# Fused attention and two-layer networks on one core: value means spread by ScalarE, a load queue that holds loads alone

## The chip, the cores and the metric

The kernel runs on one core of a Trainium2 chip. The metric is device time in microseconds (us) of one execution. Five engines run their own instruction streams beside each other and meet at semaphores: PE (TensorE, matmuls), DVE (VectorE), ACT (ScalarE), POOL (GpSimd) and SP (SyncE, which here only issues DMAs). Sixteen DMA engines move the data.

## The reference

```python
def _attn_ref(q, k, v):                      # B, H, S, D = 2, 8, 768, 64
    block, window = (32, 16)
    k_sum = k.reshape(B, H, nb, block, D).max(axis=3)
    v_sum = v.reshape(B, H, nb, block, D).mean(axis=3)
    scores_l = scale * q @ k^T, kept where |i - j| < window
    scores_s = scale * q @ k_sum^T + np.log(block)
    a = softmax(concatenate([scores_l, scores_s]))
    return a @ concatenate([v, v_sum])

def _moe_ref(x, w_in, w_out):                # 1536 tokens, 512 -> 2048 -> 512
    h = np.maximum(x @ w_in, 0.0)
    return h * h @ w_out

def _moe2_ref(x, w_in, w_out, a, b):
    h = x @ w_in
    g = (a[0] + a[1]*h + a[2]*h*h + a[3]*h*h*h) / (1.0 + |b[0]|*|h| + |b[1]|*h*h + 1e-06)
    return g @ w_out
```

Each query sees a band of 31 keys around itself and, beside them, one summary per block of 32 keys (the maximum of the keys, the mean of the values). The attention output is the input of a first network, and that one's output the input of a second.

## The kernel before

**The attention** works on eight units n = 0 to 7 (NB), each a pair of heads of one batch entry, called a head here for short. A head has 12 windows of 64 queries, done in three groups of four windows, so there are 24 groups G = 0 to 23 (GROUPS), and head n has groups 3n, 3n+1, 3n+2. For a group, PE computes the scores (`scores`, L483) against the windowed keys `kwin`; DVE adds the mask and takes the extreme (`masked`, L833, tile `prob`, `lowest`); ACT does four exponentials (`exps`, L665); DVE inverts the sums; POOL scales (`normalise`, L381); PE transposes (`turn`, L502, into bank 6); ACT copies the transposed matrix to `probT` (L687); PE multiplies with the values (`output`, L519). Scores run four groups ahead of the output, exponentials three.

**Loads per head:** queries `q` (384 KB), keys `kraw` (384 KB), windowed values `vwin` (two halves of 288 KB). DVE takes block maxima of the keys (`block_max`, L818) and POOL copies keys into windows (L351). `q`, `kraw` and `kwin` have rings of three buffers (RING), `vwin` of four (V_RING).

**Value means.** PE multiplies the values with a matrix of 1/32 (`summary(n)`, L493) in the group given by `SUMMARY_AT[n]`, ACT copies the result to `vsum` (`copy_summary`, L673), and four DMAs of 36 KB each (`spread_summary`, L262) copy the 24 means behind the 96 value rows of each of the 12 windows of `vwin`: each DMA writes 6 partitions x 12 windows of 512 B. `output(3n)` waits for all four (`vsum_in`). These DMAs read and write SBUF only.

**The queue.** Before, all loads and all spreads are issued by SP, in one written order, and each instruction that waits holds up all behind it. A load of head n+3 waits until its buffer is free; a spread waits for `vsum_copied`, that is for ACT's copy of that head's means.

**The networks** follow. PE runs them without a pause once the attention has ended: L533 (first product) and L585, L600 (second products). The weights come through `wraw` (512 KB each): three during the attention (`load_first`, split into high and low parts by POOL), the others later (`load_weights`, L272, split by DVE).

Of the kernel before, what the change touches and what calls it, by code (L numbers as in the profile page):

```python
# [28 lines left out]
P = 128  # L29
# [4 lines left out]
KW = QW + 2 * BAND  # L34
NW = S // QW
NBLK = S // BLOCK
COLS = KW + NBLK
GU = 4
GPB = NW // GU
# [9 lines left out]
FT = DF // P  # L49
# [4 lines left out]
EARLY = PAIRS - 1  # L54
# [6 lines left out]
P_RING = 4  # L61
RING = 3
V_RING = 4
NB = PAIRS * B
# [1 line left out]
KP = S + 2 * BAND  # L66
THIRD = S // GPB
SPLIT_FROM = GROUPS - 7
SUMMARY_AT = [0, 1, 3] + [GPB * n - 4 for n in range(3, NB)]


def unit(j, h):
# [4 lines left out]
def done(credits, i):  # L77

    return credits + i + 1


def build(nc, qT, kT, vw, w1, w2, coef_a, coef_b, out):
# [33 lines left out]
    ca = small("ca", [P, 4])  # L116
    braw = small("braw", [P, 2])
# [8 lines left out]
    q, kraw, kwin, vwin = [], [], [], []  # L126
# [101 lines left out]
    def landing(index, k=0):  # L228

        return (index - EARLY) % LAND, k + (index - EARLY) // LAND  # L230
# [5 lines left out]
    def _(sp):  # L236
        def load_k(n):
            if n >= RING:
                sp.wait_ge(windows_ready, GPB * (n - RING + 1))
            sp.dma_start(kraw[n % RING][:, BAND:BAND + S], kT[n]).then_inc(k_in[n % RING], 16)  # L240
# [5 lines left out]
        def load_q(n):  # L246
            if n >= RING:
                sp.wait_ge(s_done, GPB * (n - RING + 1))
            sp.dma_start(q[n % RING][:, :], qT[n]).then_inc(q_in[n % RING], 16)

        def load_vwin(n):
            if n >= V_RING:
                sp.wait_ge(o_done, done(2, GPB * (n - V_RING + 1) - 1))
            for half in (slice(0, NW // 2), slice(NW // 2, NW)):
                sp.dma_start(vwin[n % V_RING][0:KW, half, :], vw[n][:, half, :]).then_inc(vw_in[n % V_RING], 16)

        def spread_summary(n):

            sp.wait_ge(vsum_copied, n + 1)
            for t in range(4):  # L260
                rows = KW + 2 * GPB * t
                sp.dma_start(vwin[n % V_RING][rows:rows + 2 * GPB, :, :],  # L262
                             vsum[n % 2][32 * t:32 * t + 2 * GPB, :].unsqueeze(1).to_broadcast([2 * GPB, NW, P])
                             ).then_inc(vsum_in[n % V_RING], 16)

        def load_first(j):
            sp.dma_start(wraw[:, j:j + 1, :], w1[j:j + 1].rearrange("a p n -> p a n")).then_inc(w_first, 16)

        def load_weights(w, j, index, turn):
            if not (isinstance(turn, int) and turn == 0):  # L270
                sp.wait_ge(w_in[index], 16 * turn)
            sp.dma_start(wraw[:, bass.ds(j, 1), :], w[bass.ds(j, 1)].rearrange("a p n -> p a n")).then_inc(w_in[index], 16)  # L272

        load_k_first(0)
        load_k_first(2)
        load_q(0)
        load_vwin(0)
        load_k(1)
        load_q(1)
        load_k(2)  # L280
        load_vwin(1)
        load_q(2)
        for n in range(NB):
            if n == 0:
                load_vwin(2)
            elif n + RING < NB:
                load_vwin(n + RING)
            if n + RING < NB:
                load_k(n + RING)
            if n == 0:  # L290
                spread_summary(0)
                load_vwin(RING)
                spread_summary(1)
            if n + RING < NB:
                load_q(n + RING)
            if 2 <= n < 2 + EARLY:
                load_first(n - 2)
            if n == 5:
                sp.dma_start(ca[:, :], coef_a.partition_broadcast(P)).then_inc(coef_in, 16)
                sp.dma_start(braw[:, :], coef_b.partition_broadcast(P)).then_inc(coef_in, 16)  # L300
            if n >= 5:
                for j in range(EARLY + 2 * (n - 5), min(EARLY + 2 * (n - 4), FT // 2)):
                    load_weights(w1, j, *landing(j))
            if n == 1:
                spread_summary(2)
            if 0 < n and n + 2 < NB:
                spread_summary(n + 2)
        sp.wait_ge(o_done, done(2, GROUPS - 1))
        with sp.Fori(0, FT // 2 // LAND) as k:
            for i in range(LAND):  # L310
# [333 lines left out]
    def _(act):  # L644
# [13 lines left out]
            last = a.copy(means[:, j, 2 * j:2 * j + 2], mean[:, :])  # L658
        last.then_inc(means_done, 1)

        def exps(G, r):

            act.wait_ge(s_free, done(2, G))
            for u in range(GU):
                last = a.activation(prob[r][:, u, :], prob[r][:, u, :], ACT.Exp, bias=lowest[r][:, u:u + 1],  # L665
                                    scale=-1.0, accum_out=rowsum[r][:, u:u + 1])
            last.then_inc(exp_done, 1)

        def copy_summary(n):
            act.wait_ge(vsum_done, n + 1)  # L670
# [9 lines left out]
        exps(0, 0)  # L680
        exps(1, 1)
        copy_summary(0)
        exps(2, 2)
        for G in range(GROUPS):
            act.wait_ge(t_done, done(P_RING, G))
            act.wait_ge(o_done, done(2, G - 2))
            a.copy(probT[G % 2][:, :], tps[0:COLS, :]).then_inc(probT_done, 1)  # L687
            if G + 3 < GROUPS:
                exps(G + 3, (G + 3) % P_RING)
            if G == GROUPS - 2:  # L690
                relu(0, 0)
            for n in range(1, NB):
                if SUMMARY_AT[n] == G:
                    copy_summary(n)
# [352 lines left out]
```

## Time and profile before

| | |
|---|---|
| median of 3 runs | 622.24 us (619.99 to 626.68) |
| profiled execution, its own time | 619.3 us |
| its span, first to last instruction | 617.2 us |
| granted TensorE clock | 0.999 |
| last attention matmul (L519 of group 23) starts | 85.44 us |
| busy: PE, DVE, ACT, POOL | 94%, 72%, 42%, 24% of the span |

Times in the views are us from the start of the span. The span less 85.44 us is the networks, in which PE is busy throughout; the attention is the stretch ahead of it. The profiled execution's own time is 2.1 us over its span.

### The profile page before, as it was taken

The numbers are of one execution on the slowest core, as the hardware profiler recorded it, in microseconds if no ns is written. First come the engines' busy times: TensorE is split into PE (matmuls) and PEld (weight loads), VectorE is DVE, ScalarE is ACT, GpSimd is POOL, SyncE is SP. The second block draws the span as 40 slices with busy tenths as digits, with TensorE's granted clock in tenths as the row PEclk, the third lists the DMA queues.
The fourth block names the chain that finished last, engine by engine and source line by source line (L and its number), as shares of the span: only waits on it lengthen the run. The fifth ranks groups of instructions, "written<-read, shape, count | busy, mean of one in ns | idle before, by whom it ended". The sixth has DMA issues, their size and how long they took to land.

```text
span 617.2 us, 9768 instructions
## 1 busy us (share of the span) xinstructions
PE 581.2 (94%) x3360; PEld 473.0 (77%) x3360; DVE 443.0 (72%) x839; ACT 261.6 (42%) x556; POOL 147.2 (24%) x158
## 2 busy tenths in 40 slices
PE   4587899999999999999999989999999999999995
PEld 3465678888888888888888867788888888888884
DVE  5467798765343333356765699999999999999996
ACT  4477731110131110311110855566766566766564
POOL 6255640000030000120000566622222222222220
PEclk9999999999999999999999999999999999999999
DMA  8477544000000000023322200000100000100001
GB/s 252 100 212 246 191 163 184 0 1 0 1 1 0 0 0 0 0 68 103 103 102 102 69 1 0 1 0 1 68 0 0 0 0 0 69 1 0 1 1 68
DMA packets 13535, 32.55 MB, mean 53 GB/s; under 512 B 1728, under 2 KB 4416, under 8 KB 13504
## 3 DMA queue, kind: packets, MB, share of 16 engines
q1 hardware_dynamic: 13360, 31.99, 16.1%
q8 instruction: 21, 0.34, 0.2%
q10 hardware_dynamic: 144, 0.13, 0.1%
q14 instruction: 10, 0.08, 0.0%
HBM read 27.79 MB, written 3.15 MB: 50 GB/s over the span
## 4 chain that ended last, share of the span: by engine, by line
PE 46%; DVE 35%; issue 9%; ACT 3%; DMA 3%; SPq 2%; DVEq 1%; POOL 0%; POOLq 0%
PE bank L533 22%; PE bank L585 21%; DVE ratio L981 9%; DVE numer L963 6%; DVE ratio L975 5%; DVE numer L961 5%; DVE ratio L970 5%; DVE hhi L988 4%; DMA kraw<-kT 3%; ACT prob L665 2%; SPq L262 1%; PE bank L502 1%; PE bank L519 1%; DVE hlo L992 1%; PE bank L483 1%
## 5 line engine op out<-in xcount | busy, mean ns | idle before, releaser
L533 PE MATMUL bank<-xhi,whi 128*128 (+1 forms) x384 | 149.8, 390 | 0.1
L533 PE MATMUL bank<-xhi,wlo 128*128 (+1 forms) x384 | 149.4, 389 | 0.0
L533 PE MATMUL bank<-xlo,whi 128*128 (+1 forms) x384 | 149.4, 389 | 0.0
L443 POOL TENSOR_TENSOR denom<-denom,habs 128x512 f32<-128x512 f32 (+1 forms) x49 | 62.3, 1273 | 251.0 <-ACT denom L736 251.0
L678 ACT ACTIVATE hsq<-bank 128x512 f32<-128x512 f32 x48 | 28.8, 600 | 213.2 <-PE bank L533 213.1
L533 PEld LDWEIGHTS bank<-xhi,whi 128*128 128x128 f32 x384 | 72.1, 188 | 15.2 <-issue 0.3
L533 PEld LDWEIGHTS bank<-xhi,wlo 128*128 128x128 f32 x384 | 72.1, 188 | 15.1
L533 PEld LDWEIGHTS bank<-xlo,whi 128*128 128x128 f32 x384 | 72.1, 188 | 14.7
L600 PE MATMUL bank<-whi,hhi 128*128 128x512 f32 x192 | 75.9, 395 | 7.6 <-DVE hlo L992 7.6
L600 PE MATMUL bank<-wlo,hhi 128*128 128x512 f32 x192 | 74.8, 390 | 0.0
L600 PE MATMUL bank<-whi,hlo 128*128 128x512 f32 x192 | 74.8, 390 | 0.0
L585 PE MATMUL bank<-hhi,whi 128*128 128x512 f32 x192 | 74.7, 389 | 0.0
L585 PE MATMUL bank<-hlo,whi 128*128 128x512 f32 x192 | 74.7, 389 | 0.0
L585 PE MATMUL bank<-hhi,wlo 128*128 128x512 f32 x192 | 74.7, 389 | 0.0
L875 DVE TENSOR_TENSOR hsq<-hsq 128x512 f32<-128x512 f32 x48 | 33.4, 697 | 49.8 <-ACT hsq L678 49.8
L878 DVE TENSOR_SCALAR hhi<-hsq 128x512 fp32r<-128x512 f32 x48 | 21.1, 439 | 64.2 <-PE bank L585 64.1
L981 DVE SCALAR_TENSOR_TENSOR ratio<-numer,ca,ratio 128x512 f32<-128x512 f32 (+1 forms) x49 | 56.7, 1158 | 5.7
L435 POOL TENSOR_TENSOR xlo<-xraw,xhi 128x512 fp32r<-128x512 f32 x12 | 17.4, 1483 | 169.9 <-ACT xraw L713 169.9
L733 ACT ACTIVATE habs<-bank 128x512 f32<-128x512 f32 x48 | 28.8, 599 | 66.9 <-PE bank L533 51.6
L600 PEld LDWEIGHTS bank<-whi,hhi 128*128 128x128 f32 x192 | 36.0, 188 | 19.1 <-DVE hlo L992 11.8
L744 ACT ACTIVATE bank<-denom,one 128x512 f32<-128x512 f32 (+1 forms) x49 | 33.6, 686 | 32.4 <-POOL denom L443 32.4
L992 DVE TENSOR_TENSOR hlo<-ratio,hhi 128x512 fp32r<-128x512 f32 (+1 forms) x49 | 42.0, 858 | 1.7
(69 smaller groups left out, 862.2 us busy)
## 6 DMA issues: line engine op xcount, KB each, us to landing
wraw<-w SPq DMA_DIRECT2D x32, 512.0 KB, 4.1
vwin<-vw SPq DMA_DIRECT2D x16, 288.0 KB, 5.4
q<-qT SPq DMA_DIRECT2D x8, 384.0 KB, 6.0
out<-osb SPq DMA_DIRECT2D x12, 256.0 KB, 2.1
kraw<-kT SPq DMA_DIRECT2D x7, 384.0 KB, 6.1
vwin<-vsum SPq DMA_DIRECT2D x32, 36.0 KB
kraw<-kT SPq DMA_DIRECT2D x2, 128.0 KB, 2.4
kraw<-kT ACTq DMA_DIRECT2D x1, 128.0 KB, 2.7
```

Source lines behind the costliest of these rows:

```text
L443: g.tensor_tensor(denom[:, i, cols], denom[:, i, cols], habs[:, i, cols], ALU.mult).then_inc(q_done, 1)
L533: last = mm(hps[j % 2][:, :], W[a][:, j, kt * P:(kt + 1) * P], X[b][:, kt, bass.ds(CH * c, CH)], start=kt == 0 and i == 0, stop=kt == KT - ...
L585: last = mm(acc[dt][:, :], W[a][:, j, KT * P + dt * P:KT * P + (dt + 1) * P], HID[b][:, j % 2, :], start=j == 0 and i == 0, stop=j == FT - ...
L600: last = mm(acc[t][:, :], HID[a][:, j % 2, t * P:(t + 1) * P], W[b][:, j, KT * P:], start=j == 0 and i == 0, stop=j == FT - 1 and i == 2)
L744: a.activation(rcp0[bank][:, cols], denom[:, i, cols], ACT.Ln, bias=one[:, 0:1]).then_inc(ln_done, 1)
L875: d.tensor_tensor(hsq[:, i, :], hsq[:, i, :], hsq[:, i, :], ALU.mult).then_inc(sq_done, 1)
L961: d.tensor_tensor(numer[:, i, :], hps[i][:, :], numer[:, i, :], ALU.mult).then_inc(horner_done, 1)
L963: d.scalar_tensor_tensor(numer[:, i, :], numer[:, i, :], ca[:, 1:2], hps[i][:, :], ALU.subtract, ALU.mult).then_inc(h_free, 1)
L970: d.scalar_tensor_tensor(ratio[:, cols], denom[:, i, cols], one[:, 0:1], rcp0[bank][:, cols], ALU.add, ALU.mult).then_inc(t1_done, 1)
L975: d.scalar_tensor_tensor(ratio[:, cols], ratio[:, cols], -2.0, rcp0[bank][:, cols], ALU.add, ALU.mult).then_inc(t2_done, 1)
L981: d.scalar_tensor_tensor(ratio[:, cols], numer[:, i, cols], ca[:, 0:1], ratio[:, cols], ALU.subtract, ALU.mult).then_inc(ratio_done, 1)
L992: d.tensor_tensor(hlo[:, i, cols], ratio[:, cols], hhi[:, i, cols].bitcast(F32), ALU.subtract).then_inc(g_ready, 1)
```

## The change

ACT issues the spreads, one after each of the first exponentials of a group; SP issues loads only. Three things move:

- `spread_summary(n, t)` is now one DMA of ACT. Heads 0, 1 and 2 issue all four in one group of exponentials (head 0 in `exps(2)`, head 1 in those done at G = 2, head 2 at G = 5); heads 3 to 7 issue two at G = SUMMARY_AT[n] + 1 and two a group later. For heads 4 to 7 each issue also waits until the last output of the head that had the buffer is done.
- The SP queue: loads in the order q(n), k(n+1), vwin(n); the first weights behind vwin(3), vwin(4) and vwin(5); the coefficients and five more weights behind vwin(7).
- `SUMMARY_AT[2]` is 4, before 3.

```diff
-SUMMARY_AT = [0, 1, 3] + [GPB * n - 4 for n in range(3, NB)]
+SUMMARY_AT = [0, 1, 4] + [GPB * n - 4 for n in range(3, NB)]
...
         load_q(0)
+        load_k(1)
         load_vwin(0)
-        load_k(1)
-        load_q(1)
-        load_k(2)
-        load_vwin(1)
-        load_q(2)
-        for n in range(NB):
...
+        for n in range(1, NB):
+            load_q(n)
+            if n + 1 < NB:
+                load_k(n + 1)
+            load_vwin(n)
+            if RING <= n < RING + EARLY:
+                load_first(n - RING)
+        sp.dma_start(ca[:, :], coef_a.partition_broadcast(P)).then_inc(coef_in, 16)
+        sp.dma_start(braw[:, :], coef_b.partition_broadcast(P)).then_inc(coef_in, 16)
+        for j in range(EARLY, FT // 2):
+            load_weights(w1, j, *landing(j))
...
-        def exps(G, r):
+        def exps(G, r, spreads=()):
 
             act.wait_ge(s_free, done(2, G))
             for u in range(GU):
                 last = a.activation(prob[r][:, u, :], prob[r][:, u, :], ACT.Exp, bias=lowest[r][:, u:u + 1],
                                     scale=-1.0, accum_out=rowsum[r][:, u:u + 1])
-            last.then_inc(exp_done, 1)
+                if u < len(spreads):
+                    if u == GU - 1:
+                        last.then_inc(exp_done, 1)
+                    spread_summary(*spreads[u])
+            if len(spreads) < GU:
+                last.then_inc(exp_done, 1)
+
+        def spread_summary(n, t):
+
+            act.wait_ge(vsum_copied, n + 1)
+            if n >= V_RING:
+                act.wait_ge(o_done, done(2, GPB * (n - V_RING + 1) - 1))
+            rows = KW + 2 * GPB * t
+            act.dma_start(vwin[n % V_RING][rows:rows + 2 * GPB, :, :],
+                          vsum[n % 2][32 * t:32 * t + 2 * GPB, :].unsqueeze(1).to_broadcast([2 * GPB, NW, P])
+                          ).then_inc(vsum_in[n % V_RING], 16)
...
+            spreads = []
+            for n in range(1, NB):
+                first = SUMMARY_AT[n] + 1
+                if n < RING and G == first:
+                    spreads = [(n, t) for t in range(4)]
+                elif n >= RING and G == first:
+                    spreads = [(n, 0), (n, 1)]
+                elif n >= RING and G == first + 1:
+                    spreads = [(n, 2), (n, 3)]
```

On SP at the start of the program, the order as a difference. A number behind a name tells buffers apart (`kraw0`, `kraw1`, `kraw2` are the ring of keys; `vwin3` is the fourth value buffer):

```order
+L240 DMA kraw1_67<-kT 128x768
 L255 DMA vwin0_65<-vw 96x768 x2
-L240 DMA kraw1_67<-kT 128x768
...
+L240 DMA kraw0_63<-kT 128x768 [waits windows_ready]
 L255 DMA vwin2_73<-vw 96x768 x2
-L240 DMA kraw0_63<-kT 128x768 [waits windows_ready]
-L262 DMA vwin0_65<-vsum0_74 6x12x128 [waits vsum_copied]
-L262 DMA vwin0_65<-vsum0_74 6x12x128 x3
+L249 DMA q0_62<-qT 128x768 [waits s_done]
+L240 DMA kraw1_67<-kT 128x768 [waits windows_ready]
 L255 DMA vwin3_85<-vw 96x768 x2
```

The first spreads have left the queue, and the queries of head 3 and the keys of head 4 stand ahead of the values of head 3; the keys of head 4 came behind the spreads of heads 0 and 1 before.

On ACT, head 3, before:

```order
L673 COPY vsum1_75<-bank7 128x128 [waits vsum_in1,vsum_done]
L687 COPY probT0_83<-bank6 120x512 [waits o_done,t_done]
L665 ACTIVATE prob1_80,rowsum1_97<-prob1_80,lowest1_93 128x120 [waits s_free]
L665 ACTIVATE prob1_80,rowsum1_97<-prob1_80,lowest1_93 128x120 x3
L687 COPY probT1_84<-bank6 120x512 [waits o_done,t_done]
```

and the same place in the changed kernel:

```order
L661 COPY vsum1_75<-bank7 128x128 [waits vsum_in1,vsum_done]
L684 COPY probT0_83<-bank6 120x512 [waits o_done,t_done]
L638 ACTIVATE prob1_80,rowsum1_97<-prob1_80,lowest1_93 128x120 [waits s_free]
L653 DMA vwin3_85<-vsum1_75 6x12x128 [waits vsum_copied]
L638 ACTIVATE prob1_80,rowsum1_97<-prob1_80,lowest1_93 128x120
L653 DMA vwin3_85<-vsum1_75 6x12x128 [waits vsum_copied]
L638 ACTIVATE prob1_80,rowsum1_97<-prob1_80,lowest1_93 128x120 x2
L684 COPY probT1_84<-bank6 120x512 [waits o_done,t_done]
```

Two DMAs now stand between the exponentials, and two more follow in the next group.

## Rows read from the trace of the kernel before

**Rows 1.** Page, part 2: the span in 40 slices, busy tenths of PE and DMA.

```profile
PE   4587899999999999999999989999999999999995
DMA  8477544000000000023322200000100000100001
```

**Rows 2.** Waits of the SP queue, 0 to 140 us: in total, times, longest.

```profile
SPq L262 <- ACT vsum L673: 28.1, 7, 11.0
```

**Rows 3.** The chain that ended last, in order of time: start, us, what.

```profile
14.81 7.23 issue
...
26.50 0.28 ACT vsum L673
...
29.13 3.08 DMA vwin<-vsum
```

**Rows 4.** Timeline of SP: start, us, engine, line, operation.

```profile
7.43 0.40 SPq L240 DMA_DIRECT2D kraw<-kT  x1
11.49 3.27 SPq L262 DMA_DIRECT2D vwin<-vsum  x4
...
26.79 3.06 SPq L262 DMA_DIRECT2D vwin<-vsum  x4
...
31.32 0.43 SPq L240 DMA_DIRECT2D kraw<-kT  x1
...
32.27 8.66 SPq L262 DMA_DIRECT2D vwin<-vsum  x8
...
41.94 0.43 SPq L240 DMA_DIRECT2D kraw<-kT  x1
```

**Rows 5.** Timeline of DVE: the first block maxima of heads 5, 6 and 7.

```profile
47.01 0.42 DVE L818 TENSOR_REDUCE ksum<-kraw 128x8 f32<-128x256 f32 x1 [2.68 <-DMA kraw<-kT]
...
55.40 0.42 DVE L818 TENSOR_REDUCE ksum<-kraw 128x8 f32<-128x256 f32 x1 [2.18 <-DMA kraw<-kT]
...
64.14 0.42 DVE L818 TENSOR_REDUCE ksum<-kraw 128x8 f32<-128x256 f32 x1 [2.55 <-DMA kraw<-kT]
```

**Rows 6.** Timeline of PE: the outputs of groups 0, 3, 6, 18 and 23.

```profile
22.04 1.12 PE L519 MATMUL bank<-probT,vwin 120*64 120x64 f32 x16 [7.23 <-issue]
...
32.34 0.69 PE L519 MATMUL bank<-probT,vwin 120*64 120x64 f32 x16 [1.42 <-DMA vwin<-vsum]
...
39.92 0.69 PE L519 MATMUL bank<-probT,vwin 120*64 120x64 f32 x16 [1.24 <-issue]
...
72.76 0.69 PE L519 MATMUL bank<-probT,vwin 120*64 120x64 f32 x16
...
85.44 0.69 PE L519 MATMUL bank<-probT,vwin 120*64 120x64 f32 x16
```

**Rows 7.** Timeline of ACT, groups 7 to 9.

```profile
41.23 0.59 ACT L687 COPY probT<-bank 120x512 f32<-120x512 f32 x1 [0.66 <-PE bank L502]
...
42.10 0.38 ACT L665 ACTIVATE prob<-prob,lowest 128x120 f32<-128x120 f32 x1
...
43.24 0.56 ACT L687 COPY probT<-bank 120x512 f32<-120x512 f32 x1
...
45.23 0.25 ACT L673 COPY vsum<-bank 128x128 f32<-128x128 f32 x1
...
45.93 0.59 ACT L687 COPY probT<-bank 120x512 f32<-120x512 f32 x1 [0.45 <-PE bank L502]
```

**Rows 8.** Windows: length, busy PE, PEld, DVE, ACT, POOL, clock, DMA share, GB/s.

```profile
16.00:17.00 1.00, 0.00 (x0) 0.00 (x0) 0.20 (x2) 0.97 (x6) 0.00 (x0) 1.00 1.00 246
...
29.20:29.60 0.40, 0.40 (x8) 0.23 (x10) 0.14 (x2) 0.40 (x4) 0.00 (x0) 1.00 0.37 84
```

**Rows 9.** Timeline of ACT, its only DMA issue and the instruction behind it.

```profile
1.36 0.39 ACTq L653 DMA_DIRECT2D kraw<-kT  x1
1.77 1.28 ACT L654 ACT_TABLE_LOAD   x1 [1.77 <-PEq L1040]
```

**Rows 10.** Tile vwin, the spreads: duration ns min/median/max, first and last start.

```profile
L262 SPq DMA_DIRECT2D vwin<-vsum x32: 720/722/1328, 11.5 to 73.6; - x32
```

More of the change, by code:

```diff
@@ L255, in load_vwin @@
                 sp.dma_start(vwin[n % V_RING][0:KW, half, :], vw[n][:, half, :]).then_inc(vw_in[n % V_RING], 16)
[L257 to L264, printed above, removed]
         def load_first(j):
@@ L276, in _ @@
         load_q(0)
+        load_k(1)
         load_vwin(0)
-        load_k(1)
-        load_q(1)
-        load_k(2)
-        load_vwin(1)
-        load_q(2)
-        for n in range(NB):
[L284 to L307, printed above, removed]
+        for n in range(1, NB):
[9 more added lines that the diff above has]
+            load_weights(w1, j, *landing(j))
         sp.wait_ge(o_done, done(2, GROUPS - 1))
@@ L682, in _ @@
         copy_summary(0)
-        exps(2, 2)
+        exps(2, 2, [(0, t) for t in range(4)])
         for G in range(GROUPS):
+            spreads = []
[7 more added lines that the diff above has]
+                    spreads = [(n, 2), (n, 3)]
             act.wait_ge(t_done, done(P_RING, G))
@@ L688, in _ @@
             if G + 3 < GROUPS:
-                exps(G + 3, (G + 3) % P_RING)
+                exps(G + 3, (G + 3) % P_RING, spreads)
             if G == GROUPS - 2:
```

## Prediction

> **What bounds the kernel now.** I read the 40 slices first: PE is at nine tenths from the sixth slice (77 us) to the end, and the slices ahead of it have gaps, while the DMA engines are busy only in the first seven [rows 1]. The last attention output starts at 85.44 us [rows 6]; behind it PE has no pause that a load could shorten, so the change can only move the end of the attention, and everything behind moves with it one for one. Next the waits of the SP queue: SP stood 28.1 us in seven waits for ACT's copies of the means [rows 2]. The queue is in order, so what stands behind such a wait starts late. The chain of waits and the timelines then show three kinds of stall.
>
> First, PE idles 7.23 us ahead of the first output, which starts at 22.04 us [rows 3, 6]. What it waits for is `vsum_in` of head 0. Those four spreads were issued from 11.49 us on, but behind loads that went out up to 7.43 us [rows 4], and the DMA engines were full in between: share 1.00 at 246 GB/s from 16 to 17 us [rows 8].
>
> Second, output 3 waits 1.42 us and output 6 1.24 us for their spreads [rows 6]. Here nothing is queued ahead for head 1: the fourth issue starts at 29.13 us, and 3.08 us later it has landed [rows 3]. That is the latency of a spread in a quiet queue.
>
> Third, the keys: those of head 4 are issued at 31.32 us and those of head 5 at 41.94 us, each behind spreads (eight of them take SP 8.66 us from 32.27 us on) [rows 4]. DVE then waits 2.68, 2.18 and 2.55 us for the keys of heads 5, 6 and 7 [rows 5].
>
> The sum is made between outputs 0, 3, 6, 18 and 23, at 22.04, 32.34, 39.92, 72.76 and 85.44 us [rows 6].
>
> **Term a, output 0.** The four spreads go to a queue of ACT's own. Issued from 11.5 us on at 0.72 us each [rows 4, 10], the fourth starts at 13.7 us; with the 3.08 us of the quiet case [rows 3] output 0 could start at 16.8 us, a gain of 5.2, and I take 5.0 as the best. The other end: the sixteen DMA engines are the same ones, and SP's queue is fuller than before, since it holds queries 3, keys 4, values 3 and one weight beside what it held. A spread writes 72 runs of 512 B. With only spreads under way the DMA share reaches 0.37, 5.9 of 16 engines [rows 8], so I take it that four spreads put 288 / 6 = 48 runs on each of six engines. At 246 GB/s a 3 KB run of a load takes an engine 0.20 us [rows 8]. If runs of the two queues alternate one by one, 48 of them need 48 x 0.20 = 9.6 us and their own time, some 0.04 us each (84 GB/s over six engines), 1.9 us: 11.5 us, output 0 at 23.0 us, a loss of 1.0. Between +5.0 and -1.0 I take **+2.0**: no row shows both queues loaded for long, the middle is as near as the rows allow.
>
> The Trainium skill, "DMA: Bandwidth & Descriptors", section "Issuing engines are not separate DMA queues", says that DMAs started by different engines run on the same 16 DMA engines and interleave, and that issuing from several saves only the sequencer's time. By the rows the first fifteen microseconds are indeed full; by the rule taken strictly the first output would gain nothing, which is the fourth rival below.
>
> **Term b, outputs 0 to 3.** Before, 10.30 us. The means of head 1 are copied at 26.50 us, the first spread goes out at 26.79 us [rows 3, 4], 4.75 us behind output 0, and the fourth lands 5.4 us after that. ACT can issue at the same pace if its issues run beside its copy and exponentials: then 0. But before, the DMA engines had run dry at that time, and now SP has gone on to queries 4 and keys 5, 768 KB, 3.1 us at 246 GB/s [rows 8]. Between 0 and -2.5 I take **-1.0**.
>
> **Term c, outputs 3 to 6.** Before, 7.58 us. The means of head 2 are now made in group 4 instead of 3, one group (2.01 us, 41.23 to 43.24 [rows 7]) later, while `output(6)` stays where it is. Call output 3 X. Group 4's copy of the means ends at about X+3.5 (a group of 2.0, the summary's share, the copy's 0.25 [rows 7]); the next transposed copy and the first exponential follow, and the issues from X+3.7 on, the second and later ones paced at 0.77 us with the exponentials between them; the fourth starts at X+5.9 and lands at X+9.0 by the 3.08 us [rows 3]. That is 1.4 later than before; with keys and queries of later heads in the DMA engines up to 3.0. I take **-1.8**. The transposed copy of group 6 stands on ACT behind the fourth issue, but `output(6)` waits for the landing longer than for it.
>
> **Term d, outputs 6 to 18.** Before, 32.84 us for four heads, 8.21 each. Without a wait for keys a head takes 2.01 + 2.01 + 2.69 = 6.7 us: group 7 to 8 is 2.01, group 8 to 9, with a summary, 2.69 [rows 7], and in neither is there a wait for a load. Now the keys of a head are issued several groups ahead of use, since nothing but free buffers holds SP. So 4 x 6.7 = 26.8 and a gain of 6.0, if the 16 issues cost ACT nothing. ACT works 3 x 2.01 + 0.25 = 6.28 us a head [rows 7], 0.4 us of slack. One exponential is 0.38 us from start to start, an issue 0.72 and 0.05 between [rows 7, 10]; the first issue of a head can run beside the next transposed copy and exponential, the later ones while earlier work is still queued at the engine. I charge 0.2 us a head: **+5.2**. Bounds: +6.0 with nothing exposed, +3.0 if half of what exceeds an exponential shows. The landing (3.08 us) fits: the last two issues of a head come two groups ahead of its first output, and two groups take 4.0 to 4.7 us [rows 7].
>
> The Trainium skill, "Perfetto Trace Analysis", section "DVE / Act Engine Instruction", describes a wait queue and an execution FIFO between ACT's sequencer and its engine, so that a later DMA issue can run while earlier activations execute. The only ACT issue here has nothing ahead of it; what stands behind it, the table load, starts at 1.77 us, after 1.36 + 0.39 [rows 9], so an issue does hold what follows. By the rule alone nothing would be charged and d would be 6.0.
>
> **Term e, outputs 18 to 23 and on.** 12.68 us, in which PE has matmuls of the networks between; head 7's issues lie at groups 18 and 19, beside them. The weights leave SP earlier than before. Both cost **0**; without that cover two groups would take 0.4 us more each.
>
> The values of head 0 now stand behind the keys of head 1 in the queue, 384 KB, 1.6 us at 246 GB/s; the first summary waits for them, but between it and output 0 lies the idle time of term a, so nothing is charged.
>
> **Sum.** 2.0 - 1.0 - 1.8 + 5.2 + 0 = 4.4 us less. The profiled execution took 619.3 us, 2.1 over its span; it becomes 614.9. The median of the runs is 622.24, 2.9 above that execution; taking the same 4.4 off gives **617.8 us**.
>
> **Rivals.**
> 1. The second queue is served fairly well and the spreads land in 3.1 us even beside loads: a +5.0, b 0, c -1.4, d +6.0, together 9.6, **612.6 us**. For it: the quiet latency, and 512 B runs take little of an engine's time. Against it: share 1.00 where term a lies.
> 2. Slower: ACT is held by every issue and nothing overlaps. Each spread then adds 0.77 us to ACT between exponentials. The fourth issue of head 0 starts at 11.5 + 0.38 + 3 x 1.15 = 15.3 us, a +1.0; b -2.8 and c -4.2 (three pairs of 1.15 instead of 0.77, and the first issue behind the copy); d: 6.28 + 3.1 = 9.4 a head against 8.21, -4.7; e -1.3. Together -12, **634.2 us**. Its place is ACT's stream between two transposed copies; from an exposed 0.48 us per spread on (8.21 - 6.28, over four) term d turns into a loss. For it: the table load behind the one ACT issue. Against it: ACT's instructions otherwise follow each other without a gap, so they are queued ahead.
> 3. Half hidden: each issue covers only the one exponential ahead of it, 0.39 us exposed, 7.8 us a head. a +2.0, b -2.2, c -3.1, d +1.6, e -0.5: -2.2, **624.4 us**.
> 4. The change doesn't do what it says: the waits for keys are for the DMA engines, not for SP's order. Six of them carry 48 runs more per head, and a separate queue carries them on the same six. Then d is 0, a -1.0, b -1.0, c -1.8: **626.0 us**. Against it: from 29.2 to 29.6 us the DMA share is 0.37 [rows 8], with the keys of head 4 unissued until 31.32 us [rows 4].
>
> **How the numbers follow.** Forecast 0.40, first rival 0.27, second 0.12, third 0.13, fourth 0.08. The forecast's own bounds give about 613.5 to 621. The range runs from 610.0, just under the first rival, to 627.5, above the fourth; what is left out is the second rival and a little at the low end. One per cent, 6.2 us, is about what a measurement of this kernel tells from no change. Faster by more than that is the first rival and 0.07 of the forecast, 0.34; slower is the second rival and a little of the others, 0.13; within, 0.53.
>
> **What would show it.** In the changed profile: output 0 at about 20 us (16.8 in rival 1, 23 in rival 4); outputs 0 to 3 in 11.3 us, 3 to 6 in 9.4; no wait of DVE for keys past group 5; 6.7 to 6.9 us a head from output 6 to 18; ACT's exponentials in the groups with spreads 0.38 us apart where the issue is hidden, 0.77 where half hidden, 1.15 where not; no time from group 18 on. The forecast is wrong if waits for keys remain, if exponentials spread over 1.1 us, or if late spreads of heads 3 to 7 stop their first outputs, for which I charge nothing.

## The result and the profile after

The changed kernel takes **642.1 us** (median of 4 runs, 639.39 to 642.85) against 622.68 us of the kernel before beside it (4 runs): a ratio of 1.0299, 95% interval 1.0235 to 1.0362. It is slower, by some 18.5 us (the ratio times 620 us), and outside the predicted range. The profiled execution took 641.9 us, its span is 639.8 us, so 22.6 us over the span before.

The page, part 2 (40 slices, one is 16.0 us) and part 3 (queues):

```profile
PE   4356769999999999999999989999999999999996
...
PEclk9576969999999999999999999999999999999999
DMA  8645621600000000002222210000010000100001
...
q1 hardware_dynamic: 10864, 30.81, 14.6%
q10 hardware_dynamic: 2640, 1.31, 0.9%
```

PE was at 4, 5, 8, 7, 8, 9 tenths in the first six slices [rows 1] and is now at 4, 3, 5, 6, 7, 6; its granted clock, nine tenths or more in every slice before, is down in four of them. q1 is SP's queue, q10 that of ACT: the spreads moved, as the change says.

The timeline of PE, outputs of groups 0, 3, 6, 18 and 23 (start, us, engine, line, operation, idle time before and what ended it):

```profile
26.16 1.12 PE L492 MATMUL bank<-probT,vwin 120*64 120x64 f32 x16 [11.95 <-issue]
...
40.89 1.12 PE L492 MATMUL bank<-probT,vwin 120*64 120x64 f32 x16 [6.38 <-DMA vwin<-vsum]
...
54.97 1.12 PE L492 MATMUL bank<-probT,vwin 120*64 120x64 f32 x16 [5.59 <-issue]
...
94.87 0.69 PE L492 MATMUL bank<-probT,vwin 120*64 120x64 f32 x16
...
108.08 0.69 PE L492 MATMUL bank<-probT,vwin 120*64 120x64 f32 x16
```

Set against [rows 6], this gives a table in the terms of the prediction:

| stretch | before | after | difference |
|---|---|---|---|
| start to output 0 (a) | 22.04 | 26.16 | +4.12 |
| outputs 0 to 3 (b) | 10.30 | 14.73 | +4.43 |
| 3 to 6 (c) | 7.58 | 14.08 | +6.50 |
| 6 to 18 (d) | 32.84 | 39.90 | +7.06 |
| 18 to 23 (e) | 12.68 | 13.21 | +0.53 |
| after output 23 | 531.76 | 531.72 | 0.0 |

The whole loss lies in the attention, and the largest part of it is four waits of PE for spreads. Those of outputs 0, 3 and 6 were 7.23, 1.42 and 1.24 us [rows 6] and are 11.95, 6.38 and 5.59; output 15, which is shown below, did not wait and now waits 7.31. Together the waits grew by 21.3 us, against 22.6 for the span. That the two are near is partly chance: the lower clock behind the waits and ACT's issues add some microseconds, and the keys that now come in time take about as many off (both below). A wait labelled "issue" is one for which the profile names no releaser; that of outputs 0 and 6 is taken to be for the landing too, since the chain has between ACT's copy to `probT`, which ends at 16.44 us, and output 0 nothing but 9.72 us without a releaser. The last runs of ACT's queue move between 25 and 26 us, just ahead of output 0 (26.16), and between 54 and 55 us, just ahead of output 6 (54.97).

The chain that ended last (start, us, what), where it now passes through spreads:

```profile
16.44 9.72 issue
...
34.64 6.11 DMA vwin<-vsum
...
73.73 12.04 DMA vwin<-vsum
```

A spread took 3.08 us to land before [rows 3]. The fourth one of head 1 takes 6.11 us, the second of head 5's last pair 12.04. The timeline of SP tells what was in the way of the latter:

```profile
33.40 1.89 SPq L255 DMA_DIRECT2D vwin<-vw  x2
35.33 0.43 SPq L258 DMA_DIRECT2D wraw<-w  x1
...
70.14 0.78 SPq L255 DMA_DIRECT2D vwin<-vw  x2
70.96 0.43 SPq L277 DMA_DIRECT2D ca<-coef_a  x1
71.43 0.43 SPq L278 DMA_DIRECT2D braw<-coef_b  x1
71.91 38.66 SPq L263 DMA_DIRECT2D wraw<-w  x7
```

With no spread to hold it, SP issues the last values at 70.14 us and weights right behind them, and the spreads of head 5 (last two issued at 72.82 and 73.73 us) run beside them. Likewise the spreads of head 1 (32.04 to 34.64 us) run beside the values and the weight issued from 33.40 us on.

How the two queues share the DMA engines is seen in the DMA view of stretches of one microsecond (queue: runs, MB, share of 16 engines), here 15 to 16, 17 to 18, 19 to 20 and 77 to 78 us:

```profile
q1 hardware_dynamic: 101, 0.27, 106.8%
...
q1 hardware_dynamic: 86, 0.24, 93.4%
q10 hardware_dynamic: 28, 0.01, 7.8%
...
q1 hardware_dynamic: 114, 0.31, 95.1%
q10 hardware_dynamic: 41, 0.02, 7.2%
...
q1 hardware_dynamic: 101, 0.35, 99.9%
q10 hardware_dynamic: 30, 0.01, 5.0%
```

The first spread is issued at 11.82 us, yet from 15 to 16 us nothing of q10 moves: in steps of a tenth of a microsecond its first run is seen at 16.8 us. Then 23 to 41 of its runs go each microsecond, up to 24 us, when SP's thin out. The spreads lie on six of the sixteen engines (share 0.37 with nothing else under way [rows 8]), and six sixteenths of SP's 86, 114 and 101 runs are 32, 43 and 38: if SP's runs are spread evenly over the sixteen, about one small run goes for each run of 3 or 4 KB on an engine that both queues want. These are counts over a microsecond; whether single runs alternate or small groups of them is not shown. At some 30 a microsecond the 288 runs of a head take 9.6 us; 16.8 + 9.6 is 26.4, and output 0 starts at 26.16. The loads that share are of both kinds: SP had issued 4.8 MB before 11.82 us, of which 4.1 MB had moved at 16 us, and issued 1.5 MB more from 12.61 us on.

The clock in windows (length, busy PE, PEld, DVE, ACT, POOL, clock, DMA share, GB/s), 18 to 19 and 26 to 27 us:

```profile
18.00:19.00 1.00, 0.00 (x0) 0.00 (x0) 0.34 (x3) 0.59 (x4) 0.00 (x0) 0.50 1.05 284
...
26.00:27.00 1.00, 0.84 (x16) 0.87 (x16) 0.00 (x0) 0.00 (x0) 0.00 (x0) 0.50 0.05 16
```

After some microseconds without a matmul TensorE's clock went from 1.00 to 0.50, from 2.4 to 1.2 GHz, and the output that ends the wait takes 1.12 us where one at full clock takes 0.69. The timeline of PE, outputs 15 and 16, shows a whole group at the lower level:

```profile
85.90 1.12 PE L492 MATMUL bank<-probT,vwin 120*64 120x64 f32 x16 [7.31 <-DMA vwin<-vsum]
...
89.00 1.12 PE L492 MATMUL bank<-probT,vwin 120*64 120x64 f32 x16
```

3.10 us for a group that took 2.01 [rows 7]: the long waits of outputs 6 and 15 cost about one microsecond more than themselves.

What the change set out to do for the keys it did: DVE has no wait for `kraw` left in the first 110 us (2.68, 2.18 and 2.55 us before [rows 5]).

### The profile page after: what moved, and what is told of

Its sections match the earlier page's. It is cut to its first block, busy times and chain, and to the rows that moved or that the text cites. A ratio compares the mean times of both kernels' runs of the same rounds, so it can differ in the third digit from the quotient of the medians.

```text
span 639.8 us, 9784 instructions
## 1 busy us (share of the span) xinstructions
PE 587.5 (92%) x3360; PEld 478.1 (75%) x3360; DVE 443.0 (69%) x839; ACT 263.1 (41%) x556; POOL 147.5 (23%) x158
## 3 DMA queue, kind: packets, MB, share of 16 engines
q1 hardware_dynamic: 10864, 30.81, 14.6%
## 4 chain that ended last, share of the span: by engine, by line
PE 48%; DVE 33%; issue 10%; DMA 3%; ACT 3%; DVEq 1%; ACTq 1%; POOL 0%; POOLq 0%
PE bank L506 21%; PE bank L558 20%; DVE ratio L978 9%; DVE numer L960 5%; DVE ratio L972 5%; DVE numer L958 5%; DVE ratio L967 5%; DVE hhi L985 3%; DMA vwin<-vsum 3%; PE bank L492 2%; PE bank L475 2%; PE bank L456 1%; PE bank L466 1%; ACTq L653 1%; ACT prob L638 1%
## 5 line engine op out<-in xcount | busy, mean ns | idle before, releaser
L492 PE MATMUL bank<-probT,vwin 120*64 120x64 f32 x384 | 19.1, 251 | 33.7 <-issue 17.5
```

Of the source, the lines that this page charges most:

```text
L492: last = mm(ops[k % 2][rows, cols], vwin[r][:, GU * gi + u, D * h:D * h + D], probT[par][:, first:first + QW], start=True, stop=True)
```

## Experiments

The ratio is always to the kernel before, run on the same chip beside it. "Time" is the median of the runs. The gain or loss in brackets is the ratio times 620 us, so that kernels of different chips can be set side by side; that of the changed kernel is +18.5 us. Its own interval is wide, 14.6 to 22.4 us by the same rule.

| run | time, us | ratio (95% interval) | about |
|---|---|---|---|
| e1_issuer_only | 629.46 | 1.0133 (1.0100 to 1.0166) | +8.2 |
| e2_loads_between | 619.25 | 0.9966 (0.9931 to 1.0001) | -2.1 |
| e3_hold_weights | 634.84 | 1.0224 (1.0190 to 1.0259) | +13.9 |
| e4_one_dma | 632.61 | 1.0188 (1.0156 to 1.0219) | +11.7 |
| e5_gate_on_landing | 626.03 | 1.0082 (1.0052 to 1.0111) | +5.1 |
| e6_summary_early | 635.79 | 1.0230 (1.0197 to 1.0263) | +14.3 |
| e7_keys_ahead | 619.37 | 0.9980 (0.9957 to 1.0003) | -1.2 |
| e8_keys_ahead_start | 619.76 | 0.9975 (0.9952 to 0.9998) | -1.6 |
| e9_order_by_hand | 615.27 | 0.9907 (0.9873 to 0.9942) | -5.8 |
| e10_small_on_act | 631.80 | 1.0154 (1.0115 to 1.0193) | +9.5 |

The theory after the result (**sharing**): a spread in a queue of its own loses its place in the line; whatever SP has still under way, issued before it or behind it, shares the engines with it, about run for run. Rivals: ACT's issuing costs ACT's time (**issue**), and SP's new order alone is at fault (**order**).

### e1: only the issuer changed

The kernel before, SP's order as it was, and SP still waits for the copied means where the spread stood; the four DMAs are issued by ACT at the changed kernel's places, but for head 2, whose means and spreads come one group earlier, since `SUMMARY_AT[2]` is 3 as before.

```diff
         def spread_summary(n):                    # SP
             sp.wait_ge(vsum_copied, n + 1)
-            for t in range(4):
-                sp.dma_start(vwin[...], vsum[...])
+                if u < len(spreads):              # ACT, in exps
+                    spread_summary(*spreads[u])
```

> The kernel before, with the spreads issued by ACT exactly where the changed kernel issues them; SP keeps its old order of loads and its old waits for the copied means, so that loads are released when they were before. Sharing theory (the 512 B runs of ACT's queue take turns one for one with the 3 to 4 KB runs of SP's queue on the six DMA engines that carry spreads, so the loads behind a spread now run beside it): output 0 at 24 to 26 us, 2 to 4 later than before; output 3 waits 4 to 6 us instead of 1.4; in all 628 to 638 us. Issue theory (what the change costs is ACT's time, some 0.4 us shown per issue): output 0 within 1 us of before, some 2 to 4 us longer in all, 624 to 627. Order theory (the new order of the load queue costs the time): as before, 622.

629.46 us, +8.2. Outputs 0 and 3:

```profile
23.02 1.12 PE L514 MATMUL bank<-probT,vwin 120*64 120x64 f32 x16 [8.30 <-issue]
...
37.94 1.12 PE L514 MATMUL bank<-probT,vwin 120*64 120x64 f32 x16 [6.34 <-DMA vwin<-vsum]
```

Output 0 is 1.0 us later than before, which is no more than profiles differ by: it starts at 20.86 us in e7 and at 22.87 us in e10, whose SP orders are the same up to there. So it meets the issue theory's expectation (within 1 us) and misses the sharing theory's (24 to 26 us). Output 3 is 5.6 us later, with a wait of 6.34 instead of 1.42, and outputs 9 and 15, which did not wait before, wait 3.34 and 2.05 us. SP's order is that of before, but it is no longer held while the four issues run, so the loads that stood behind a spread now run beside it. The total lies in the sharing theory's 628 to 638 us, and above the issue theory's 624 to 627. Order alone is not the fault: almost half the loss is there without it. ACT waits 6.2 us in all for its issues here, so a part of the 8.2 us may be theirs; this run does not tell the two apart. From 18 to 19 us q10 moves 31 runs against SP's 100, six sixteenths of which are 38.

### e2: one queue, the loads spread evenly between the spreads

Everything on SP. For each head n: spread n, keys n+3, values n+2, queries n+3; the first keys go ahead of the first values.

```diff
         for n in range(NB):
+            spread_summary(n)
+            if n + 3 < NB:
+                load_k(n + 3)
+            if n + 2 < NB:
+                load_vwin(n + 2)
+            if n + 3 < NB:
+                load_q(n + 3)
```

> The kernel before with its issuer (SP) kept and the loads put in order of use between the spreads: keys n+3, values n+2, queries n+3 behind the spread of head n, one queue for all. Sharing theory: in one queue nothing issued later can pass a spread, and keys are early enough; output 0 at 17 to 18 us, no wait for keys, 611 to 616 us. Order theory: it is the order of the loads that costs, 630 or more. Issue theory: ACT does not issue, so no loss, 611 to 622.

619.25 us: a gain that the interval does not separate from none, short of what was expected. Output 0 starts at 19.2 us instead of 22.0 and DVE no longer waits for keys, but outputs 9 and 12 now wait 1.94 and 2.34 us for spreads. Their spreads now stand in the one queue right behind loads; that of head 3, for one, behind keys, values, queries and a weight, all issued from 33.07 to 36.44 us.

### e3: the late weights held back

The changed kernel, and SP waits for output 21 before it issues the last weights.

```diff
+        sp.wait_ge(o_done, done(2, GROUPS - 3))
         for j in range(EARLY, FT // 2):
             load_weights(w1, j, *landing(j))
```

> The changed kernel with one wait more on SP: the five weight loads behind the values of head 7 start only when output 21, the last first output of a head, is done. Sharing theory: output 15 no longer stops for 7.3 us, everything ahead of it stays, 633 to 636 us. Issue and order theories: the wait at output 15 has another cause and stays, 641 to 643.

634.84 us, +13.9 against +18.5; the two intervals overlap a little, so the size of the gain is uncertain. Output 15:

```profile
79.31 0.69 PE L493 MATMUL bank<-probT,vwin 120*64 120x64 f32 x16
```

Its wait of 7.31 us is gone, and nothing else changed in the source; so it was the weights that made the spreads late. The networks did not pay for the later weights: from output 23 to the end it is 532.9 us against 531.7, and 532.9 also in e4 and e6, whose weights come early. The expectation of the sharing theory held.

This run also gives the price of ACT's issues free of waits for spreads. From output 6 on nothing waits for a spread, and a head takes 7.3 us instead of the 6.7 that the prediction built on [rows 7]. ACT's timeline, groups 9 to 11:

```profile
64.00 0.58 ACT L685 COPY probT<-bank 120x512 f32<-120x512 f32 x1 [0.65 <-PE bank L476]
64.06 0.75 ACTq L654 DMA_DIRECT2D vwin<-vsum  x1
64.48 0.40 ACT L639 ACTIVATE prob<-prob,lowest 128x120 f32<-128x120 f32 x1
...
64.97 0.75 ACTq L654 DMA_DIRECT2D vwin<-vsum  x1
...
65.77 0.40 ACT L639 ACTIVATE prob<-prob,lowest 128x120 f32<-128x120 f32 x1 [0.41 <-issue]
...
66.54 0.56 ACT L685 COPY probT<-bank 120x512 f32<-120x512 f32 x1
66.97 0.80 ACTq L654 DMA_DIRECT2D vwin<-vsum  x1
...
68.60 0.56 ACT L685 COPY probT<-bank 120x512 f32<-120x512 f32 x1
...
71.32 0.58 ACT L685 COPY probT<-bank 120x512 f32<-120x512 f32 x1 [0.49 <-PE bank L476]
```

The first issue (64.06 us) runs beside the copy and costs nothing. The second covers one exponential, and the next starts 0.41 us late, right behind the issue's end at 65.72. The group lasts 64.00 to 66.54, 2.54 us against 2.01 [rows 7]; the next, with its issues, 2.06; the third, 2.72 against 2.69. That is 7.32 a head, 0.58 of it from issuing.

### e4: one DMA for each head, on twelve engines

The changed kernel with the 24 means in 24 adjacent partitions, so that one DMA of 288 runs replaces four. For that the matrix of 1/32 is [96, 12, 32] and the summary is 12 matmuls in one accumulation.

```diff
-            rows = KW + 2 * GPB * t
-            act.dma_start(vwin[...][rows:rows + 2 * GPB, :, :], vsum[...][32 * t:32 * t + 2 * GPB, :] ...)
+            act.dma_start(vwin[...][KW:COLS, :, :], vsum[...][0:NBLK, :] ...)
...
+            for w in range(NW):
+                last = mm(vps[0:32, 0:P], means[:, w, :], vwin[n % V_RING][0:KW, w, :],
+                          start=w == 0, stop=w == NW - 1)
```

> The changed kernel with the 24 means of a head in 24 neighbouring partitions (twelve matmuls into one set of 32 rows instead of four sets), so that one DMA of ACT's with 24 partitions does the work of four with 6. The bytes and the 288 runs of 512 B stay; if the partitions decide how many DMA engines share a DMA, twelve carry them instead of six. Sharing theory: 24 runs an engine instead of 48, the waits at outputs 0, 3, 6 and 15 about half as long, 624 to 631 us. Issue theory: 24 issues fewer, 0.36 us each at most, 633 to 639, with the waits at the outputs unchanged from landing on.

632.61 us, +11.7. Outputs 0 and 3, and the summary:

```profile
26.78 1.12 PE L491 MATMUL bank<-probT,vwin 120*64 120x64 f32 x16 [10.32 <-issue]
...
37.81 0.69 PE L491 MATMUL bank<-probT,vwin 120*64 120x64 f32 x16 [0.57 <-DMA vwin<-vsum]
...
39.58 2.81 PE L465 MATMUL bank<-vwin,means 96*32 96x128 f32 x24
```

The time lies between the two expectations. The waits of outputs 3, 6 and 15 are 0.57, 0 and 0, with SP's order and its early weights unchanged; a part of that is the longer summary, which delays everything else too. With nothing else under way the share of q10 now reaches 64% (36.4 to 36.6 us), so more than six engines carry it. The DMA view of 22 to 23 us shows the rate beside loads:

```profile
q1 hardware_dynamic: 81, 0.24, 88.7%
q10 hardware_dynamic: 60, 0.03, 17.7%
```

Twelve sixteenths of 81 are 61: run for run again, at twice the rate, if 24 partitions mean twelve engines. That is the clearest sign for the sharing theory. But the summary in this form takes 2.81 us instead of 0.86 (ACT waits 14.6 us for it, over the eight heads), which eats the gain; and output 0 is no earlier, because the issue, at 15.22 us, moves its first run at 20.2 us. That delay of 5.0 us is as long as in the changed kernel (11.82 to 16.8), and more engines do not shorten it.

### e5: SP waits until spreads have landed

The changed kernel; SP waits for the landing of spread n-2 before it issues what comes after head n's loads, so that few loads run beside a spread. The weights behind the coefficients wait in the same way for the spreads of heads 6 and 7.

```diff
+        def landed(n):
+            sp.wait_ge(vsum_in[n % V_RING], 64 * (n // V_RING + 1))
...
+            landed(n - 2)
```

> The changed kernel (ACT issues, new order of loads) with waits on SP: behind the queries of head 2 it waits until the spreads of head 0 have landed, behind the values of head 3 for those of head 1, then for those of each further head, before it issues loads again; so few loads run beside spreads. Sharing theory: the waits at outputs 0, 3, 6 and 15 shrink to 1 to 6 us, 1 to 2, 1 to 2 and none; output 0 at 18 to 20 us; 612 to 622 us. Issue theory: ACT still issues all 32, so 632 or more.

626.03 us, +5.1: between the two expectations. The waits of outputs 0, 3 and 6 are 3.84, 3.34 and 2.29 us, output 15 does not wait, but outputs 9 and 12, which did not wait in the changed kernel, wait 1.55 and 3.89. From this run's waits:

```profile
ACT prob L657 <- issue: 6.4, 15, 1.1
```

ACT is held by issues as long as in the changed kernel, so the 13.4 us that the gate gave back are not ACT's. What stays has both parts in it, since the gated loads now come later and outputs still wait.

### e6: the summary of head 2 at group 3, as before

```diff
-SUMMARY_AT = [0, 1, 4] + ...
+SUMMARY_AT = [0, 1, 3] + ...
```

> The changed kernel with the means of head 2 made in group 3 again instead of 4, and its four issues one group earlier. Position theory: the wait at output 6 (5.6 us) falls by one group, 2 us or more, 638 to 640 us. Sharing theory: as much, if the loads that take turns with this spread are the same; if they are the weights behind the values of head 4 as well, nothing is gained, 638 to 643.

635.79 us, +14.3. The wait of output 6 falls from 5.59 to 1.67 us, and outputs 3 to 6 take 9.75 us instead of 14.08: the one group of delay was worth about four microseconds. The medians say the same (14.3 against 18.5), though their intervals overlap. Both expectations asked for less. That a spread in shared engines needs about twice the lead of the quiet latency would explain it, but this is argued. This profile also shows how much the start varies: output 0 starts at 30.10 us here and at 27.69 in e3, against 26.16, with the same source up to there.

### e7 and e8: the kernel before, keys ahead of the spread

e7 issues the keys of head 4 and later ahead of the spread they stood behind; e8 also puts spread 0 ahead of values 2 and keys 3.

```diff
             if n == 1:
                 spread_summary(2)
+            if n + 1 + RING < NB:
+                load_k(n + 1 + RING)
             if 0 < n and n + 2 < NB:
                 spread_summary(n + 2)
```

> The kernel before, SP issuing everything, with one thing moved: from head 4 on the keys stand ahead of the spread behind which they stood. Order reading (the keys waited for SP's order): DVE's waits of 2.68, 2.18 and 2.55 us for keys go, outputs 6 to 18 take 28 instead of 32.8 us, 615 to 618 us. Bandwidth reading (they waited for DMA engines): the waits stay or turn into waits for spreads that land later, 620 to 624.

> The same, and at the start the values of head 2 and the keys of head 3 stand behind the spread of head 0, the values of head 3 behind that of head 1. If output 0 waits for what is queued ahead of its spreads, it starts at 18 to 19 us instead of 22.0, and the total is 2 to 4 us under the kernel with the keys alone, 611 to 615 us; if not, the same as that one.

619.37 and 619.76 us: -1.2, which the interval does not separate from none, and -1.6, which it barely does; the 611 to 615 us expected of e8 are missed. In e7 the three waits of [rows 5] are gone, one for keys is left, 0.88 us long, and output 23 starts at 83.4 instead of 85.4 us. So the waits for keys do come from SP's order, and one queue can cure them. In e8 output 0 starts at 17.1 us, 4.9 earlier, the place in the line being worth nearly what the prediction called its best; but output 6 then waits 3.05 us, its spread being behind 2.3 MB of loads issued after that of head 1, 0.6 MB more than in e7, and DVE waits 2.97 us for keys at 59.95 us. The first microseconds are only lent.

In e7 PE also stopped in the middle of one group's matmuls, with all operands of the group ready (e2, e8 and e9 show such stops too, of 1.29, 1.34 and 0.57 us):

```profile
62.27 0.39 PE L520 MATMUL bank<-probT,vwin 120*64 120x64 f32 x5
...
64.40 0.57 PE L520 MATMUL bank<-probT,vwin 120*64 120x64 f32 x11 [1.74 <-issue]
```

Weights were issued at 63.44 us. That its instructions came late through full DMA engines is an argument, not shown.

### e9: one queue, an order written for every spread

Everything on SP. The first spread stands ahead of values 2; for heads 3 to 5 each spread n-2 has keys n, values n-1 and queries n ahead of it, and a weight behind it.

```diff
+        spread_summary(0)
+        load_vwin(2)
+        load_k(3)
+        load_q(3)
+        load_k(4)
+        load_vwin(3)
+        spread_summary(1)
+        load_q(4)
+        spread_summary(2)
+        for n in range(5, NB):
+            load_k(n)
+            load_vwin(n - 1)
+            load_q(n)
+            spread_summary(n - 2)
+            load_first(n - 5)
...
+        spread_summary(6)
+        for j in range(EARLY, FT // 2 - 1):
+            load_weights(w1, j, *landing(j))
+        spread_summary(7)
```

> SP issues everything in one queue, in an order written by hand so that little is queued ahead of a spread and SP is never idle with free buffers: values 2, keys 3, queries 3, keys 4, values 3 between the spreads of heads 0 and 1 (SP stood idle there for six microseconds), queries 4 ahead of the spread of head 2, then per head keys, values of the head before, queries, spread. If one queue with the right neighbours is what counts: output 0 at 17 us, output 3 at 27, output 6 at 34 to 35, then 7.4 a head, 610 to 615 us. If the loads issued ahead delay the spreads of heads 1 and 2 as they did in the two kernels with the keys ahead: 617 to 621.

615.27 us (613.79 to 616.45), ratio 0.9907: 0.9% faster than the kernel before, and so faster than both. Outputs 0, 3, 15 and 23:

```profile
17.97 1.12 PE L517 MATMUL bank<-probT,vwin 120*64 120x64 f32 x16 [3.29 <-issue]
...
28.29 0.69 PE L517 MATMUL bank<-probT,vwin 120*64 120x64 f32 x16 [0.32 <-DMA vwin<-vsum]
...
60.38 0.69 PE L517 MATMUL bank<-probT,vwin 120*64 120x64 f32 x16 [0.74 <-DMA vwin<-vsum]
...
79.98 0.69 PE L517 MATMUL bank<-probT,vwin 120*64 120x64 f32 x16
```

Output 23 starts 5.5 us before that of [rows 6]. The two goals of the change, early first spread and keys in time, are had from the order alone. Output 0 and output 6 (34.74 us) come about when expected; a head then takes 8.0 us, not the expected 7.4, and the total is just above the 610 to 615 us.

### e10: ACT's issues, nearly without bytes

The kernel before, and beside its own spreads (SP's) ACT issues 32 DMAs of 2 KB (128 runs of 16 B each, into a tile that nobody reads) at the changed kernel's places. This adds work; it leaves nothing out.

```diff
+            act.wait_ge(vsum_copied, n + 1)
+            act.dma_start(junk[:, 4 * i:4 * i + 4], coef_a.partition_broadcast(P))
```

> The kernel before with 32 small DMAs more, issued by ACT at the places where the changed kernel issues the spreads (each copies the four coefficients to 128 partitions of an unused tile, 2 KB). The spreads stay on SP and nothing waits for the small ones until the attention is over. It prices ACT's issuing alone. Issue theory: 5 us or more over before. Sharing theory: the issues hide beside exponentials but for some tenths, 0 to 3 us over before.

631.80 us, +9.5. The time is what the issue theory asked for, but not by its mechanism: ACT lost almost nothing to these issues, and the loads came late. From the waits of this run:

```profile
ACT prob L667 <- issue: 0.9, 3, 0.5
...
DVE ksum L841 <- DMA kraw<-kT: 13.9, 4, 6.0
```

An issue here takes 0.33 to 0.39 us and hides beside an exponential, so it is no test of the 0.75 us ones. But 64 KB in all, in 4,096 tiny runs, raised the longest wait for keys from 2.7 to 6.0 us and that of output 3 from 1.42 to 4.29. Nor is it the sharing of busy engines. From 47 to 50 us the DMA share is 0.11 at 28 GB/s, although SP has issued values, keys, queries and a weight from 46.05 us on: the engines are mostly idle, some 60 to 70 runs of q10 go by each microsecond, and the loads hardly move. These runs differ from spreads in two ways, their size and their source, for each reads the same 16 B of `coef_a` in memory; the run doesn't tell which of the two it is. The two loads of coefficients, of the same kind, leave such a hole in the kernel before as well, in one queue: SP issues them at 65.67 and 66.17 us, and from 67 to 69 us the DMA share is 0.10 and 0.09. So e10 says little of spreads.

The run shows one thing of ACT's stream. An issue behind an exponential that waits for DVE does not go ahead of it:

```profile
56.30 0.39 ACT L667 ACTIVATE prob<-prob,lowest 128x120 f32<-128x120 f32 x1 [4.69 <-DVE lowest L856]
56.31 0.34 ACTq L680 DMA_DIRECT2D junk<-coef_a  x1
```

## Why the prediction was wrong

**The place was right, the sign was not.** PE's waits at the outputs 0, 3, 6 and the keys' waits decide, and everything behind output 23 moved with it one for one (531.76 and 531.72 us). The forecast priced the spreads by the landing of a quiet queue where the changed kernel has none.

**Term a (+2.0 taken, -4.1 measured; bounds +5.0 and -1.0).** The step that failed is the choice of the middle, and the lower bound. The arithmetic of that bound, runs of the two queues one by one, was the mechanism: it gave some 11.5 us for 288 runs, and from the first of them to output 0 it was 9.4 (16.8 to 26.16). What it lacked is the time before the first run, 5.0 us (11.82 to 16.8), which no row of before could show, since no second queue was loaded there.

**Terms b and c (-1.0 and -1.8 taken, -4.4 and -6.5 measured).** Their bounds charged other traffic by its bytes, 768 KB or 3.1 us, or nearly nothing. The measured landing of 6.11 us fits a price per run of the second queue better than one per byte ahead. Term c also let the summary slip by a group at 1.4 to 3.0 us; e6 puts that step at about four.

**Term d (+5.2 taken, -7.1 measured).** Three pieces. "The landing (3.08 us) fits" failed for head 5: 12.04 us, a wait of 7.31 and one microsecond of half clock. Without it (e3) the stretch takes 30.8 us, a gain of 2.0. Second, ACT: 0.2 us a head was charged, 0.58 measured in e3, so 1.5 us over four heads; the prediction's bound "half of what exceeds an exponential shows" was nearer. Third, one group at half clock behind output 6's wait, 1.1 us. 26.8 + 4 x 0.6 + 1.1 gives 30.3, against 30.8. The gain from the keys was real. The lower clock behind a wait was in no term at all.

**Term e (0 taken, -0.5 measured).** The step "The weights leave SP earlier than before. Both cost 0" failed, not in its own stretch but in term d's: e3 shows that these weights stopped output 15. Cover was looked for on PE and ACT, not on the DMA engines, where the moved loads went.

**The rivals.** The first (fair second queue) is what failed most clearly. The second came within 8 us of the time by luck, for its mechanism was not at work: ACT waited 5.9 us in all for issues, not 0.77 for each, and e5 keeps that wait while it gives back 13.4 us. The third's 0.39 us exposed by an issue is what ACT shows (0.41), in one of two issues or fewer. The fourth had the right place, the same six engines, but took away gains only; it did not let a spread that had been in time become late, and e7 refutes its claim on the keys.

The Trainium skill, "DMA: Bandwidth & Descriptors", section "Issuing engines are not separate DMA queues", says that DMAs of different issuers run on the same sixteen engines and interleave, with only the issuing time saved. Engines and interleaving are as the DMA view shows (30 against 38 runs on six engines). The prediction drew from it that the first output would be left where it was. In e1, which changes the issuer alone, that is so within what profiles differ by (1.0 us), but output 3 is 5.6 us later, and in the changed kernel the first output is 4.1 us later. That issuing from a second engine can lose time, the page does not say.

**Parts and sum.** Issuer alone +8.2 (e1). The changed order puts another 10.3 on top. Holding back the late weights takes 4.6 off (e3), head 2's summary in its old group 4.2 (e6); each of the two is hardly clear of the noise as a time, but shows in its trace as the wait that is gone. That they add up with e1 was not tried in one kernel.

**The bounds.** The recorded "613.5 to 621" is not what the terms' own bounds add up to. With all of them at the good end the gain is 9.6 us, 612.6; with all at the bad end it is a loss of 3.5, 625.7. Either way the result lies outside.

**Open.** Why the second queue's first run comes 5.0 us after the issue (in e1 5.8, in e4 5.0) when the first is deeply loaded, and 1.4 us after it when it is not (32.04 to 33.4 us). Why from 74 to 76 us hardly a run of q10 moves although two spreads are under way and SP's share is 11% in the first of these microseconds: that stretch is some two microseconds of output 15's wait in which the engines were not busy. It comes right behind the two coefficient loads, like that of 67 to 69 us in the kernel before; in e3 the same loads have no weights behind them, and 137 runs of q10 go from 75 to 76 us. And what stops PE within a group in e7.

## What to carry to other kernels

A small transfer that someone waits for is worth most in the queue in which its place can be chosen: in a queue of its own it is no longer behind the loads, but shares each engine about run for run with what is still under way, also with loads that had stood behind it. Before a queue is relieved of waits, ask what it will issue sooner and beside what; a wait that looks like waste may be what keeps the engines clear. A latency read where nothing else ran is no price for a place where something does, and a stall that idles TensorE for some microseconds costs about one more in clock.

## What had not been expected of the hardware

- Two loaded DMA queues moved about equal counts of runs on an engine, 512 B against 3 to 4 KB: 30 to 38 on six engines, 60 to 61 on what is taken for twelve (e4).
- With the first queue full, the second's first run came 5.0, 5.8 and 5.0 us after the issue (changed kernel, e1, e4); with little in it, 1.4 us after.
- 64 KB in runs of 16 B, all of the same 16 B of memory, cost 9.5 us in a second queue, and the DMA engines were mostly idle meanwhile (e10, 47 to 50 us, 0.11).
- ACT's issue of a spread takes 0.75 us (1.37 the first time) and covers a copy or one exponential; what exceeds it shows, 0.41 us. ACT's sequencer runs ahead of work under way, but not past an instruction that waits (56.30 and 56.31 us in e10).
- The summary's matmuls (96*32 on 96x128, x24) took 2.81 us as one accumulation in one bank region (e4), 0.86 us as four side by side.
